# A fourth pair of cosine and sine tiles in the first stage, and an earlier, evenly spread split of the up-weight in the second mixing

## The reference

```python
kv = np.einsum('bhsd,bhse->bhde', k, v)
out = np.einsum('bhsd,bhde->bhse', q, kv)
x = out / rms(out) * g_norm                    # 8 heads of 64 -> 512 channels
theta = x @ w_theta
zr, zi = x * np.cos(theta), x * np.sin(theta)
u = x + w_tok_r @ zr + w_tok_i @ zi            # mixes the 576 tokens
x2 = u + np.maximum(u @ w_ch, 0.0)
h = np.maximum(x2.T @ w_tok1, 0.0) @ w_tok2    # "second mixing", over tokens
u2 = x2 + h.T
out = u2 + np.maximum(u2 @ w_ch1, 0.0) @ w_ch2
```

## Time and profile before

| what | us |
|---|---|
| median of 3 runs (lowest, highest) | 1243.74 (1241.02, 1243.75) |
| the profiled execution, whole | 1244.14 |
| its span from first to last instruction | 1242.3 |
| PE busy in the span | 1193.6 (96%) |
| DVE, ACT, POOL busy | 822.1, 502.9, 366.5 |
| mean granted TensorE clock | 0.992 of full |

### The profile page before, as it was taken

The page is one execution under the profiler, slowest core; times in us unless marked ns, Lnnn a source line. Parts: engine busy times, 40 slices in busy tenths (PEclk is TensorE's granted clock), DMA queues, the critical chain, the costliest instruction groups (busy, mean ns, idle before and its releaser), DMA issues.

```text
span 1242.3 us, 20595 instructions
## 1 busy us (share of the span) xinstructions
PE 1193.6 (96%) x7590; PEld 1156.4 (93%) x7590; DVE 822.1 (66%) x1220; ACT 502.9 (40%) x796; POOL 366.5 (29%) x216
## 2 busy tenths in 40 slices
PE   6989999999999999989989999999999989999998
PEld 5789999989999999979978999999999889999998
DVE  2877767676766767666666566677766676666664
ACT  3533424252433324242333345555555533333331
POOL 3442534444253435440273133033112420000000
PEclk9999999999999999989999999999999999999999
DMA  9825436272444440054988677847659999989982
GB/s 241 172 47 113 80 83 107 38 150 40 104 69 93 76 102 12 29 127 156 294 294 300 198 285 269 300 193 282 254 199 339 365 320 287 271 240 296 278 193 51
DMA packets 348428, 228.12 MB, mean 184 GB/s; under 512 B 268880, under 2 KB 316368, under 8 KB 347344
## 3 DMA queue, kind: packets, MB, share of 16 engines
q1 hardware_dynamic: 348368, 227.32, 63.4%
HBM read 136.84 MB, written 92.80 MB: 185 GB/s over the span
## 4 chain that ended last, share of the span: by engine, by line
PE 65%; issue 13%; DVE 8%; POOL 4%; DMA 3%; SPq 3%; ACT 2%; DVEq 0%; POOLq 0%; ACTq 0%
PE bank L42 12%; PE bank L43 12%; PE bank L44 12%; PE bank L1225 9%; PE bank L1226 9%; PE bank L1227 9%; PE bank L257 2%; DVE weights_fraction L626 1%; SPq L166 1%; POOL z_z L809 1%; DVE tokens_cos L623 1%; DMA weights_down<-w_scratch 1%; PE bank L245 1%; DMA weights_raw_u<-u_scratch 1%; POOL z_z L811 1%
## 5 line engine op out<-in xcount | busy, mean ns | idle before, releaser
L42 PE MATMUL bank<-weights_tok,z_z 128*128 128x288 f32 x576 | 175.8, 305 | 14.7 <-ACT z_z L476 9.2
L43 PE MATMUL bank<-weights_tok,z_z 128*128 128x288 f32 x576 | 171.6, 298 | 0.0
L44 PE MATMUL bank<-weights_tok,z_z 128*128 128x288 f32 x576 | 171.5, 298 | 0.0
L42 PEld LDWEIGHTS bank<-weights_tok,z_z 128*128 128x128 f32 x576 | 110.0, 191 | 18.2 <-ACT z_z L476 10.6
L43 PEld LDWEIGHTS bank<-weights_tok,z_z 128*128 128x128 f32 x576 | 110.1, 191 | 0.0
L44 PEld LDWEIGHTS bank<-weights_tok,z_z 128*128 128x128 f32 x576 | 109.9, 191 | 0.0
L794 POOL TENSOR_TENSOR weights_rms_inverse<-weights_mean_squares,weights_minus_half 128x8 f32<-128x8 f32 x40 | 65.5, 1638 | 140.3 <-DVE weights_mean_squares L593 140.1
L809 POOL TENSOR_TENSOR z_z<-tokens_cos,z_z 128x512 fp32r<-128x512 f32 x32 | 51.3, 1604 | 177.7 <-ACT z_z L476 176.9
L483 ACT ACTIVATE weights_x_channel_major<-attention_u 128x288 fp32r<-128x288 f32 x64 | 28.4, 444 | 152.2 <-DVE attention_u L655 152.2
L42 PE MATMUL bank<-weights_x_channel_major,weights_ch 128*128 128x288 f32 x256 | 77.2, 301 | 0.0
L653 DVE TENSOR_TENSOR attention_u<-bank,weights_x_channel_major 128x288 f32<-128x288 f32 x64 | 29.1, 455 | 70.3 <-PE bank L44 69.5
(11 more groups left out here) (274 smaller groups left out, 3687.7 us busy)
## 6 DMA issues: line engine op xcount, KB each, us to landing
g_scratch<-attention_staged SPq DMA_DIRECT2D x36, 960.0 KB, 4.5
weights_g<-g_scratch SPq DMA_DIRECT2D x24, 1152.0 KB, 8.7
g_scratch<-attention_staged SPq DMA_DIRECT2D x36, 384.0 KB, 4.7
x_scratch<-attention_u SPq DMA_DIRECT2D x8, 1152.0 KB, 4.5
u_scratch<-attention_u SPq DMA_DIRECT2D x8, 1152.0 KB, 6.6
weights_raw_u<-u_scratch SPq DMA_DIRECT2D x6, 1536.0 KB, 8.9
qkv_u_left<-u_scratch SPq DMA_DIRECT2D x12, 768.0 KB, 9.8
qkv_k<-in_k_dram SPq DMA_DIRECT2D x32, 256.0 KB, 4.9
```

Of the source, the lines that this page charges most:

```text
L42: eng.matmul(out, w[0], x[0], start=first, stop=False)
L43: eng.matmul(out, w[0], x[1], start=False, stop=False)
L44: return eng.matmul(out, w[1], x[0], start=False, stop=last)
```

## The change

In the first stage tile 3 gets tiles of its own, `cos_tile[3]` and `sin_tile[3]`, which are the two tiles of `xn`; tile 4 goes back to slot 0. So `fraction` and `sines` of tile 3 wait for no z any more, and those of tile 4 wait for z of tile 0 instead of 1. `norm` of the next batch's rows 0 and 1 gets a wait for POOL's `z_lo` of tile 3. On ACT `z_hi` of tile 0 moves ahead of `sines` of tile 1, and in batch 0 `z_hi` of tile 2 ahead of `sines` of tile 3; on DVE in batch 0 `rotate` of tile 3 moves ahead of `fraction` of tile 4.

In the second mixing `up_lo` steps 0 and 1 move from batch 1 to batch 0, step 2 to batch 1 behind the first sum, step 4 behind the tokens of batch 4, and the two sums after it stay behind those of batch 2; ACT's `up_hi` steps move with them. SP loads x2 of batch 0 in `load_second` instead of `load_first`, x2 of batch 1 behind the tokens of batch 1, both remaining weight quarters in batch 0 behind the store of u2, and issues `store_last_turned` 2 and 3 one batch later.

```diff
     frac, sin_t, cos_t = m["fraction"], m["sin"], m["cos"]
+
+    cos_tile = [cos_t[:, 0, :], cos_t[:, 1, :], cos_t[:, 2, :], xn[:, 0, :], cos_t[:, 0, :]]
+    sin_tile = [sin_t[:, 0, :], sin_t[:, 1, :], sin_t[:, 2, :], xn[:, 1, :], sin_t[:, 0, :]]
...
@@ -457,12 +460,12 @@
 
             m, i = rows(j), j % 2
             act.wait_ge(d_frac, NT * b + j + 1)
-            done = NK * b + 2 * max(j - 2, 0)
+            done = NK * b + 2 * max(j - NJ + 1, 0)
             wait(act, a_zhi, done)
             wait(act, g_zlo, done)
-            act.activation(sin_t[0:m, j % 3, :], frac[0:m, i, :], ACT.Sin, scale=TWO_PI).then_inc(a_sin, 1)
+            act.activation(sin_tile[j][0:m, :], frac[0:m, i, :], ACT.Sin, scale=TWO_PI).then_inc(a_sin, 1)
...
@@ -535,17 +538,19 @@
                 act.wait_ge(d_wlo, 2)
                 for j in range(NT):
                     z_hi(0, j)
-                    if 1 <= j <= 2:
-                        sines(0, j + 2)
+                    if j >= 2 and j + 1 < NT:
+                        sines(0, j + 1)
                 act.wait_ge(s_raw[2], DMA)
                 act.activation(wch[0][:, :, :], raw_ch[:, :, :], ACT.Copy).then_inc(a_whi, 1)
             else:
                 for j in range(NT + 2):
                     if j < NT:
                         turn(b, j)
+                    if j == 2:
+                        z_hi(b, 0)
                     if 1 <= j <= NT:
                         sines(b, j - 1)
-                    if j >= 2:
+                    if j >= 3:
                         z_hi(b, j - 2)
...
@@ -596,6 +601,8 @@
             i = j % 2
             dve.wait_ge(g_pow, NT * n + j + 1)
             wait(dve, g_x, NT * n + max(j - 1, 0))
+            if j < 2:
+                wait(dve, g_zlo, NK * n - 1)
             dve.tensor_tensor(xn[:, i, :].rearrange("p (h e) -> p h e", h=H),
...
@@ -617,20 +624,20 @@
                 dve.scalar_tensor_tensor(out=frac[0:m, i, :], in0=ps_theta[j][0:m, :], scalar=1.0 / TWO_PI,
                                          in1=frac[0:m, i, :], op0=ALU.mult, op1=ALU.add).then_inc(d_turns, 1)
                 dve.wait_ge(d_turns, b + 1)
-            done = NK * b + 2 * max(j - 2, 0)
+            done = NK * b + 2 * max(j - NJ + 1, 0)
             wait(dve, a_zhi, done)
             wait(dve, g_zlo, done)
-            dve.tensor_scalar(cos_t[0:m, j % 3, :], frac[0:m, i, :], ROUND, ROUND, ALU.add,
+            dve.tensor_scalar(cos_tile[j][0:m, :], frac[0:m, i, :], ROUND, ROUND, ALU.add,
...
         def rotate(b, j):
@@ -638,9 +645,9 @@
 
             m, i = rows(j), j % 2
             dve.wait_ge(a_sin, 2 * (NT * b + j + 1))
-            dve.tensor_tensor(cos_t[0:m, j % 3, :], cos_t[0:m, j % 3, :], xtm[0:m, j, :], ALU.mult).then_inc(d_z, 1)
-            zi = sin_t[:, j % 3, :] if j < NJ else cos_t[LEFT:P, j % 3, :]
-            dve.tensor_tensor(zi, sin_t[0:m, j % 3, :], xtm[0:m, j, :], ALU.mult).then_inc(d_z, 1)
+            dve.tensor_tensor(cos_tile[j][0:m, :], cos_tile[j][0:m, :], xtm[0:m, j, :], ALU.mult).then_inc(d_z, 1)
+            zi = sin_tile[j][:, :] if j < NJ else cos_tile[j][LEFT:P, :]
+            dve.tensor_tensor(zi, sin_tile[j][0:m, :], xtm[0:m, j, :], ALU.mult).then_inc(d_z, 1)
...
@@ -733,8 +740,7 @@
                 for j in range(3, NT):
                     fraction(0, j)
                     magnitude(0, j)
-                rotate(0, 3)
-                rotate(0, 4)
+                    rotate(0, j)
...
@@ -930,7 +936,6 @@
         sp.wait_ge(*prev["p_out"])
         sp.wait_ge(*prev["g_x"])
         sp.wait_ge(*prev["stored_but_last"])
-        load(sp, 0, 0)
...
@@ -940,10 +945,11 @@
         sp.wait_ge(*prev["p_theta"])
         sp.wait_ge(*prev["turned_but_last"])
         load_tokens(sp, 0)
-        load(sp, 1, 1)
+        load(sp, 0, 0)
         load_quarter(sp, 0, 0)
         load_quarter(sp, 0, 1)
         load_tokens(sp, 1)
+        load(sp, 1, 1)
 
...
@@ -954,17 +960,17 @@
                     sp.wait_ge(*prev["stored"])
                     sp.wait_ge(*prev["turned"])
                 load_tokens(sp, n + 2)
-            if n == 1:
+            sp.wait_ge(d_u, NG * (n + 1))
+            sp.dma_start(u2_dram[:, :, n * S:(n + 1) * S], u2[:, :, :]).then_inc(s_st, DMA)
+            if n == 0:
                 sp.wait_ge(*prev["d_x2"])
                 load_quarter(sp, 1, 0)
-            sp.wait_ge(d_u, NG * (n + 1))
-            sp.dma_start(u2_dram[:, :, n * S:(n + 1) * S], u2[:, :, :]).then_inc(s_st, DMA)
+                load_quarter(sp, 1, 1)
             if n + 2 < B:
                 load(sp, n % 2, n + 2)
-            if n == 0:
+            if n == 1:
                 store_last_turned(sp, 2)
-            if n == 1:
-                load_quarter(sp, 1, 1)
+            if n == 2:
                 store_last_turned(sp, 3)
             if n == B - 4:
                 sp.wait_ge(g_w, len(UP_ORDER))
@@ -1140,7 +1146,7 @@
...
-    UP_BATCH = [1, 1, 2, 2, 3, 3, 4]
+    UP_BATCH = [0, 0, 1, 2, 3, 3, 4]
...
         a11, a12, a21, a22 = raw_up
-        behind_tokens(1)
+        behind_tokens(0)
         up_lo(0)
         up_lo(1)
+        behind_tokens(1)
         gp.wait_ge(s_up[2], DMA)
         add(up_sum, a11, a21, ALU.subtract)
+        up_lo(2)
         behind_tokens(2)
-        up_lo(2)
         gp.wait_ge(g_sum, 1)
         add(a21, a21, a22, ALU.add)
         gp.wait_ge(g_sum, 2)
@@ -1189,8 +1196,8 @@
         up_lo(3)
         gp.wait_ge(g_sum, 3)
         add(a12, a12, a11, ALU.subtract)
+        behind_tokens(4)
         up_lo(4)
-        behind_tokens(4)
         up_lo(5)
         up_lo(6)
```

18 lines of the change are left out of this document (9 added, 9 removed).

## The result

The changed kernel takes 1237.19 us (median of 7 runs, 1235.98 to 1238.75), the kernel before took 1243.38 us in the same comparison (7 runs, 1239.06 to 1244.15). The ratio is 0.9959, with a 95% interval of 0.9945 to 0.9974: 5.1 us faster, between 3.2 and 6.8. 1226.5 was forecast, with 1217 to 1237 as the range: the sign was right, the gain was a third of the forecast, and the median lies 0.2 us outside the range.

The account below looks back on a forecast made before the run. TensorE is busy nearly throughout, so only its waits, for late z in the first stage and freed banks in the second mixing, could pay: 6.0 + 4.0 + 2.4 + 4.9 = 17.3 us off 1244.1, given as 1226.5 us, range 1217 to 1237.

Parts of the forecast that it names:

- Batch 0: First stage, batch 0: about 1.4 us of loss left and no slow clock, 4.0 us gained, between 2.5 and 5.4.
- Steady batches: First stage, six batches: about 0.3 of 1.3 us lost stays, 1.0 gained a batch, 6.0 in all; bounds 0 to 1.3 each.
- the lay-out: First stage, batch 2 in the new order: POOL's lower part of tile 2 on time, tile 3's at 209.0, wanted at 208.9.
- rival A: First stage: DVE and POOL turns take the gain back, steady batches gain nothing, batches 0 and 7 half; 1236 us, chance 0.16.
- ACT's new order: First stage: z_hi of tile 0 ahead of tile 1's sines ends those about 1.0 us later, lets POOL begin at 192.1.
- Batch 7: First stage, last batch: smaller waits replace one of 3.84 us with the slow clock behind it; 2.4 us gained, bounds 0 and 5.
- the half clock only behind single waits of over 3 us: PE's clock, first stage: rows show half clock only after such waits; otherwise batch 7 would gain 1 instead of 2.9 us.
- POOL's order: Second mixing: two POOL operations fit each of batches 0 to 3 without collision, all 7.6 us gone; batch 4's third costs 1.2.
- the late load of u: Second mixing's end: the third stage's load of u is freed about 3 us later against the batches, costing 1.0 us (0 to 3).
- The collision in batch 5: Second mixing: batch 4's third POOL operation laps over by 1.5 us, slowing one token subtraction in batch 5; costs about 1.2 us.
- Load of x2 of batch 0 moves behind the tokens: Second mixing, DMA: with batch 1's load, 1.18 MB more ahead of the last x2 store, 3.0 us of queue; costs 0.5 us.
- Rival B: Second mixing transfers: tokens up to 2 us late twice, load of u 3 us late, no gain there; 1231.3 us, chance 0.12.

Follow-up runs that it names:

- the run above: Changed kernel with x2 of batch 0 loaded in two pieces, plus 24 already-met waits in DVE's program ahead of the first stage's loop: 1235.09 us, ratio 0.9934.
- the old loads: Kernel before with only the second mixing changed, x2 loads of batches 0 and 1 at their old places: 1235.75 us, ratio 0.9941.

## Why the prediction was wrong

**Batch 0.** Right in mechanism, 3.0 instead of 4.0: PE's long wait is gone, the granted clock is 1.00 from 57 to 78 us, as said, and the 1.28 us ahead of the first step lie in what the text allowed. But 1.5 of the 3.0 are the half clock of the earlier trace rows's execution, which another trace of the same first stage doesn't have (17.50 above), so that part of the agreement is luck.

**Steady batches: the step that failed** is the lay-out with "each instruction at its duration alone and DVE and POOL in turns". Up to `fraction` of tile 3 it holds: POOL begins 7.1 us ahead of PE's first step (7.2 forecast), `fraction` of tile 3 3.5 ahead, as forecast. Then DVE's two products of tile 2 were to end 0.2 us behind the first step (199.5 for 199.27) and end 1.45 behind it (195.98 for 194.53), because each takes 1.76 us and not 0.68, in turns one by one; POOL's lower part of tile 2 ends 7.2 us behind instead of 6.2. With 0.18 instead of 1.0 us a batch the lower bound that I had named ("0 a batch if DVE's and POOL's turns shift everything by 1 us") was what came, and rival A described it. The evidence was in the rows that I quoted, 1.40 us for what takes 0.43 alone, and I counted it as a fact of the old order instead of a price of overlap. The old order's wait of 2.49 us was the time in which POOL ran undisturbed; filling it moves the work under POOL. Cutting POOL's work, or DVE's, frees PE (67.39, 67.50); moving it gives or costs little (68.37, 69.25).

**ACT's new order** was counted as part of the gain, and costs 0.23 us a batch.

**Batch 7.** 0.16 instead of 2.4. Two steps failed. A block of DVE's code comes late there, 2.24 us of idle, for which the old order had cover: it waits 2.51 us for POOL ahead of tile 3 of that batch.

```profile
539.98 1.40 DVE L623 TENSOR_SCALAR tokens_cos<-weights_fraction 128x512 f32<-128x512 f32 x1 [2.51 <-POOL z_z L811]
```

No row of before showed it. And "the half clock only behind single waits of over 3 us" was a rule drawn from one case: 2.45 us brought it in the run above. The ports and ACT's order act here as in the steady batches: 69.77 without most of the idle time, 69.13 with ACT's old order, 67.26 with the magnitudes on ACT. These are single traces, and the clock alone moves batch 7 by 1.2 to 1.4 us, so only the last is clear by itself.

**Second mixing.** The terms of POOL's order and of the late load of u held in sum (7.6 - 1.2 - 1.0 = 5.4 forecast, 5.5 measured with the old loads). The collision in batch 5 came as forecast (its period is 13.82, 1.1 over, for 1.2). The late load of u cost 0.4 at most (the last period is 13.14) for 1.0, and 0.8 us in the first and third periods, for which I had no term, made up for it; so far the sum was luck. The step that failed is "Load of x2 of batch 0 moves behind the tokens ...; 0.5 us (0 to 2)": it costs 4 us (6.5 against 2.3, and 7.3 against 3.3). The last stores are issued later and more slowly, and the tokens of batch 2 stand behind them on SP. Rival B had priced the tokens at 2 us twice. I had also read this load's move as a choice of order, and missed that the new tile forces it: the gain of one half had to be set against the cost in the other.

**Chances and range.** "Faster" was right. Rival A (1236) and rival B (1231.3) were each held to come alone, at 0.16 and 0.12; both came together, or nearly so (0.9 us in the steady batches and 0.5 in the second mixing), and no case of mine added them. The ends of the range should have been built from two failures at once.

## What to carry to other kernels

When an engine's wait is filled with work, ask what ran undisturbed in that wait: if it shares ports with the work that moves in, the gain is the idle time less the overlap price of each pair, here 1.07 us for each POOL operation beside DVE. Take work off the shared ports before reordering it. When a tile reuses memory, look at which transfer loses its early start, and count what stands behind that transfer's queue. And where an engine idles for nothing that the profile shows in code outside a loop, look at the DMA queue of instructions, and shift the code by a few met waits: ten such waits took 4 us off one stage here.

## What the runs showed of the hardware that I had not expected

- **Turns are taken for each instruction, also by products of two SBUF operands.** DVE's 128x512 product takes 0.69 us alone and 1.76 beside POOL, a POOL subtraction of the same size 1.27 and up to 2.66. The Trainium skill (SBUF — State Buffer, Who interferes with whom) says that whoever issues first holds the ports for that whole instruction; the traces agree, 1.76 being 0.69 and most of a POOL operation.
- **Code outside a loop can come late.** DVE or ACT idle 2.1 to 3.9 us at one place of their program, up to some 2 us behind a packet of the queue of instructions. DVE's was longer with more bulk loads under way (3.57 with 0.88 MB more in front, 0.31 with the weights' loads held back). That the packet is what they wait for is inferred: the gap goes with the place in the program and ends behind the packet, but the profile names no cause. The Trainium skill (Runtime: NRT & Kernel Launch, Instruction fetch mechanics) calls the crossing into a new block mostly hidden, and a taken branch what breaks the fetching ahead; both places lie behind the engine's loop, and there it wasn't hidden.
- **The clock does not go by one wait's length.** In the run with 24 waits on DVE a wait of 2.45 us brought 1.2 GHz at once, one of 2.68 us eleven us later did not:

```profile
535.00:539.00 4.00, 3.66 (x17) 3.69 (x18) 3.93 (x6) 2.93 (x6) 2.19 (x3) 0.57 0.98 321
546.00:550.00 4.00, 3.66 (x26) 3.49 (x27) 2.40 (x2) 0.87 (x2) 3.87 (x4) 1.00 0.00 0
550.00:554.00 4.00, 4.00 (x32) 4.00 (x32) 0.43 (x1) 0.00 (x0) 0.83 (x1) 1.00 0.02 4
```

The columns are the stretch, its length, busy time of PE, PEld, DVE, ACT and POOL with the number of instructions, the granted clock (1.00 is 2.4 GHz), and DMA. So the rule of 3 us in my prediction doesn't hold, and the runs don't show which other one does. Nor does the same wait in the same code bring the same: 3.34 us in batch 0 did in two traces and not in a third (the result section), and 2.56 us in batch 7 left the clock at 1.00 in the run with the magnitudes on ACT, while 2.57 in the one with x2 in two pieces besides brought 0.50 from 534 to 540 us. The Trainium skill (TensorE: Matmul & The Clock Gate, Part 1) lets the clock go by how busy PE has lately been; that speaks against my rule too, and these rows don't decide more.
- **SP itself is slow to issue stores behind bulk loads**: four stores of the turned x2 took 4.2 to 5.1 us with as many bytes in front as in the kernel before, 5.2 with 0.3 MB more, and 7.4 to 8.2 with 1.2 MB more.
